# A joined row of block a placed one group sooner on VectorE, and three pieces of split weights moved, in a fused attention and two-layer kernel

## The reference

```
for t in range(S):                      # batch 4, 8 heads, S = 768, D = 48
    cur = einsum(u * k[t], v[t])
    y[t] = einsum(r[t], state + cur)
    state = w[t][..., None] * state + einsum(k[t], v[t])
x = rows of y as 3072 tokens x 384
xn = x / sqrt(mean(x*x) + 1e-6) * rms_g
x1 = (silu(xn @ w_gate) * (xn @ w_val)) @ w_out          # 384 -> 1536 -> 384
out = (s * relu(x1 @ w_in)**2 + b) @ w_out2              # 384 -> 2048 -> 384
```

## Time and profile before

| | |
|---|---|
| time, median of 3 runs | 1005.98 us (1005.86 to 1006.84) |
| the profiled execution | 1004.6 us, of which the span from first to last instruction is 1002.8 us |
| busy, of the span | PE 98%, DVE 56%, ACT 33%, POOL 27% |
| granted TensorE clock | mean 0.985; 1.00 of full speed in the stretch from 60 us to 604 us |
| stage 1 | about 60 us to 160 us of the span |
| stages 2 to 5 | about 94 us each, 160 us to 540 us |

### The profile page before, as it was taken

How to read it: one execution, slowest core, us unless ns; L and a number is a source line. 1 busy time by engine, 2 the same in 40 slices (tenths; PEclk the granted TensorE clock), 3 DMA queues, 4 the chain that set the end, 5 groups by cost and what they waited for, 6 DMA issues and landing times.

```text
span 1002.8 us, 23059 instructions
## 1 busy us (share of the span) xinstructions
PE 982.6 (98%) x9704; PEld 818.8 (82%) x9704; DVE 560.8 (56%) x783; ACT 331.9 (33%) x570; POOL 270.9 (27%) x199
## 2 busy tenths in 40 slices
PE   7888999999999999999999999999999999999998
PEld 7877788888888878888888888888888888888898
DVE  7799967774866487558743225506236054161440
ACT  1452324233323323242323445405225053160340
POOL 4654624362644346234600650000000000000000
PEclk7799999999999999999999999999999999999999
DMA  7380243117013601440126201021020110201000
GB/s 283 111 330 3 91 148 111 38 56 226 33 50 104 198 2 49 159 142 3 49 62 233 69 16 64 1 32 32 11 52 0 21 42 10 52 0 21 12 8 24
DMA packets 70779, 73.97 MB, mean 74 GB/s; under 512 B 50465, under 2 KB 55073, under 8 KB 69409
## 3 DMA queue, kind: packets, MB, share of 16 engines
q1 hardware_dynamic: 70112, 71.52, 22.5%
q10 hardware_dynamic: 576, 1.14, 0.3%
HBM read 59.27 MB, written 13.37 MB: 72 GB/s over the span
## 4 chain that ended last, share of the span: by engine, by line
PE 85%; DVE 9%; issue 4%; ACT 1%; POOL 0%; DMA 0%; DVEq 0%; ACTq 0%; POOLq 0%
PE value_o_ps L676 12%; PE mix_gate_ps L676 12%; PE o_ps L1598 11%; PE level_ps L47 10%; PE o_ps L688 8%; PE mix_gate_ps L1598 5%; PE mix_gate_ps L47 5%; PE value_o_ps L47 5%; PE value_o_ps L688 4%; DVE K L1035 3%; PE level_ps L624 2%; PE mix_gate_ps L624 2%; PE o_ps L1611 2%; PE level_ps L511 2%; DVE near L1075 2%
## 5 line engine op out<-in xcount | busy, mean ns | idle before, releaser
L1372 POOL TENSOR_TENSOR R<-R,arena 128x512 f32<-128x512 f32 x72 | 110.3, 1545 | 179.1 <-PE level_ps L511 81.8
L1697 DVE SCALAR_TENSOR_TENSOR sqr<-relu,sb_col 128x512 f32<-128x512 f32 x96 | 72.3, 753 | 73.2 <-ACT relu L1659 73.2
L1214 DVE TENSOR_TENSOR u_raw<-value_o_ps,u_raw 128x512 f32<-128x512 f32 x66 | 45.4, 688 | 98.6 <-PE value_o_ps L676 98.6
L909 ACT ACTIVATE u_hi<-u_raw 128x512 fp32r<-128x512 f32 x66 | 41.7, 632 | 163.6 <-DVE u_raw L1214 163.6
L902 ACT ACTIVATE u_raw<-mix_gate_ps 128x512 f32<-128x512 f32 x72 | 43.0, 597 | 146.7 <-PE mix_gate_ps L676 146.7
L676 PE MATMUL mix_gate_ps<-x_hi,w_hi 128*128 128x512 f32 x216 | 85.4, 396 | 0.5 <-DVE w_lo L1199 0.5
L676 PE MATMUL value_o_ps<-x_hi,w_hi 128*128 128x512 f32 x216 | 85.8, 397 | 0.0
L676 PE MATMUL value_o_ps<-x_hi,w_lo 128*128 128x512 f32 x216 | 84.2, 390 | 0.0
L676 PE MATMUL mix_gate_ps<-x_hi,w_lo 128*128 128x512 f32 x216 | 84.2, 390 | 0.0
L676 PE MATMUL mix_gate_ps<-x_lo,w_hi 128*128 128x512 f32 x216 | 84.2, 390 | 0.0
L676 PE MATMUL value_o_ps<-x_lo,w_hi 128*128 128x512 f32 x216 | 84.1, 389 | 0.0
(11 more groups left out here) (221 smaller groups left out, 2351.4 us busy)
## 6 DMA issues: line engine op xcount, KB each, us to landing
kr_nat<-kr SPq DMA_DIRECT2D x10, 1152.0 KB, 5.8
K<-kT SPq DMA_DIRECT2D x12, 512.0 KB, 4.3
arena<-wT SPq DMA_DIRECT2D x12, 512.0 KB, 6.3
R<-rT SPq DMA_DIRECT2D x10, 512.0 KB, 3.9
w_raw<-wgv SPq DMA_DIRECT2D x12, 384.0 KB, 5.4
v_sb<-v SPq DMA_DIRECT2D x12, 384.0 KB, 4.3
x_scratch<-x_sb SPq DMA_DIRECT2D x18, 256.0 KB, 2.3
x_raw<-x_scratch SPq DMA_DIRECT2D x6, 768.0 KB, 4.5
```

The lines of the kernel that those rows point to most:

```text
L1214: dve.tensor_tensor(u[:, f % 2], value_ps[:], u[:, f % 2], ALU.mult).then_inc(u_done, 1)
L1372: pool.tensor_tensor(q, q, decay(blk, l, 0), ALU.mult).then_inc(rmul_done, 1)
L1697: dve.scalar_tensor_tensor(out=sq[f % 2][:], in0=relu[f % 2][:], scalar=sb_col[:, 0:1], in1=relu[f % 2][:], op0=ALU.mult, op1=ALU.mult).th ...
```

## The change

The tables change, and one use of them. The placing of block a's joined middle row on DVE gets its own table and moves from behind group 7 to behind group 6 in all stages from 1 on. PE's table is not changed. Of stage 1's split weights, wo_lo piece 1 moves from group 7 to 6, and w_lo of f = 8 from group 17 to 19. Because the tables are read in a fixed order inside one group, u_lo of f = 2 now stands behind the moved work.

```
 LOWER_AT, MIDDLE_AT = (3, 5), (7, 9)
+MIDDLE_PLACED_AT = (6, 9)
...
-LATE_WEIGHTS = (5, 8, 9, 11, 14, 17, 20, 23, 28)
-LATE_OUT = (7, 13, 16, 25, 27)
+LATE_WEIGHTS = (5, 8, 9, 11, 14, 19, 20, 23, 28)
+LATE_OUT = (6, 13, 16, 25, 27)
...
-            if k in MIDDLE_AT:
-                blk = MIDDLE_AT.index(k)
+            if k in MIDDLE_PLACED_AT:
+                blk = MIDDLE_PLACED_AT.index(k)
                 place_middle(s, blk)
                 advance_third(s, blk)
```

## The result

| | before | changed |
|---|---|---|
| median of 12 runs | 1006.04 us (1003.1 to 1007.78) | 1003.81 us (1002.17 to 1004.82) |
| ratio to before | | 0.9978, 95% interval 0.9970 to 0.9986 |
| profiled execution | 1004.6 us, span 1002.8 | 1003.75 us, span 1002.0 |

The account below looks back on a forecast made before the run. PE is busy almost throughout, so DVE's order is worth at most PE's 4.8 us of waits. -1.1 + 0 - 0.7 = -1.8 us takes 1005.98 to 1004.2 us; own range 1003.8 to 1004.7, 8 in 10 from 1003.0 to 1005.9 us.

Parts of the forecast that it names:

- Stages 2 to 5: Sooner copies of block a's middle row end PE's wait at the joined matmuls: 0.27 us a stage, -1.1 us.
- the idle bracket: PE's idle time shown for the copy wait in stages 2 to 5: 0.21 us a stage, the lower bound.
- Stage 1, groups 6 and 7: DVE and POOL take turns, so the new order ends at the same 87.6 us: 0 us.
- the copy wait: PE's wait for block a's middle row; its 0.34 us piece before `out 2` becomes more wait for u_lo.
- w_lo, -0.7 us: Moving w_lo of f = 8 ends PE's 0.76 us keys wait in stage 1; first `attend` starts 0.7 us sooner.
- The idle in stage 1: Rival: DVE's 0.76 us idle in groups 6 and 7 comes back; -2.6 us, 1003.4 us, chance 0.19.
- the later stages: Rival: stages 2 to 5 give nothing, another wait ending just behind the copies; -0.7 us, 1005.3 us, chance 0.12.
- second turn: Rival: POOL takes two turns in a row ahead of stage 1's u_lo; -0.1 us, 1005.9 us, chance 0.07.
- the states were not made late: Rival denied here: moved w_lo makes stage 1's state sums late; +0.3 us, 1006.3 us, chance 0.07.
- the first rival: DVE's 0.76 us idle in stage 1 comes back, `out 2` starts sooner; 1003.4 us, chance 0.19.

Follow-up runs that it names:

- the part alone: Changed kernel with w_lo of f = 8 back at group 17: distance 525.95 us, 1.10 us less than before, ratio 0.9985.
- w_lo alone: Kernel before with only w_lo of f = 8 moved from group 17 to 19: distance 526.27 us, 0.78 us less, ratio 0.9997.
- POOL held: Changed kernel with POOL's three natural products of stage 1 kept back until DVE has made w_lo of f = 4: distance 523.39 us, ratio 0.9953.
- the states first: Changed kernel with w_lo of f = 9 and 10 made behind the state sums: 526.90 us, ratio 0.9989; run again 524.81 us.
- the old order with POOL held: Kernel before with POOL's three natural products of stage 1 kept back until DVE has made w_lo of f = 4: distance 527.17 us, one run.
- The filled wait: Changed kernel with identity matmuls, results unused, where PE waits at `out 2` in stage 1: distance 529.39 us, ratio 1.0038.

## Why the prediction came out as it did

The forecast was 1004.2 us, and 1003.81 us was measured. The forecast difference was 1.8 us. The distance shows 1.87 us, the timed runs 2.2 us (1.4 to 3.0). By its steps:

- **Stages 2 to 5, -1.1 us.** Right. The distance between joined matmuls fell from 5.67 to 5.39 us, and the part alone gives 1.10 us. Taking the difference of distances (0.27 us) and not the idle bracket (0.21 us) was worth 0.2 us of accuracy. u_lo had 1.7 us of slack, as worked out.
- **Stage 1, groups 6 and 7, 0 us.** Right, and for the reason given. The key quarter, wo_lo and u_lo end 0.28, 0.82 and 0.55 us behind POOL's instructions, where I had 0.30, 0.81 and 0.54 us. `out 2` starts 7.22 us behind u (7.30 us before), gate 4 still waits 0.5 us, and the bracket at `out 2` grew by the 0.3 us of the copy wait. With POOL's three products away, the same change of order makes wo_lo and u_lo ready 1.1 us sooner.
- **w_lo, -0.7 us.** The amount is right, and partly by luck: the first `attend` starts 47.07 us behind u, before 47.76 us, so 0.69 us. The path is right, since the state sum is what `attend` then starts behind, but two terms were off by 0.2 us and cancel. I had the state sum 0.26 us later, and it is 0.07 us later (46.86 against 46.79 us). w_lo did end 0.82 us behind POOL, where I had 0.81 us, but POOL's products began some 0.2 us sooner than I had them. And I let `attend` start at the very end of the sum. It starts 0.21 us behind it (47.07 against 46.86 us), and 0.20 us behind it with w_lo alone and with POOL held. That the state sum set the start is shown by the run with the states first, where the sum ends 1.0 us sooner and `attend` starts 0.27 us sooner.
- **Rivals.** The idle in stage 1 did not come back, the later stages gave what they should, POOL took no second turn, and the states were not made late. With POOL's products out of the way the idle does come back, as the first rival has it.
- **The chances.** I gave 0.59 to less than 0.2% and 0.35 to more. The ratio of 0.9978 is just beyond, with an interval over both, so this is not decided. The span forecast for the profiled execution (1001.0 us) missed by 1.0 us because stage 0 was longer in it.

## What to carry to other kernels

An idle stretch on the engine that is waited for is worth filling only when what it delays would not have been held anyway. Here, in groups 6 and 7 of stage 1, each VectorE instruction with two SBUF inputs was held to the end of a GpSimd instruction, and swapping them permuted the turns and saved nothing. Beside VectorE instructions that read PSUM, GpSimd work cost VectorE nothing, so place the two by what they read. Measure a gain of 1 to 2 us in 1000 by the distance between two events in the traces, with the parts alone adding up to the whole, before believing a median of runs that spread by 3 us or more. Look at the granted clock inside the distance first, since one fall of it was worth more than the whole change.

## What the runs showed of the hardware

In the first execution with the states first, PE stood idle for 2.59 us at `out 2`, and the clock it was then granted was 0.50 (1.2 GHz), against 1.00 (2.4 GHz) before. Its matmuls of 512 columns started 0.43 us apart instead of 0.23 us. In order of time:

```profile
87.86 0.80 PE L689 MATMUL o_ps<-u_hi,wo_hi 128*128 128x512 f32 x1 [2.59 <-DVE u_lo L1223]
88.46 0.63 PE L689 MATMUL o_ps<-u_lo,wo_hi 128*128 128x512 f32 x1
88.89 0.63 PE L689 MATMUL o_ps<-u_hi,wo_lo 128*128 128x512 f32 x1
```

The same happened in the old order with POOL held, behind an idle of 2.08 us, where the fall is seen after the second matmul:

```profile
96.73 0.50 PE L688 MATMUL o_ps<-u_hi,wo_hi 128*128 128x512 f32 x1 [2.08 <-DVE u_lo L1222]
...
97.36 0.63 PE L688 MATMUL o_ps<-u_hi,wo_lo 128*128 128x512 f32 x1
```

It did not happen behind the 2.27 us of the earlier trace rows, nor behind the 2.2 and 2.3 us of the two parts alone, nor behind the 2.6 and 2.5 us of the two executions of the changed kernel and the 2.6 us of the second one with the states first. So the same program has it in one execution and not in another, and it costs 2.1 us in the distance (526.90 against 524.81 us). The Trainium skill (TensorE: Matmul & The Clock Gate, Part 1: The HAM clock gate) says that a gate sets the engine's clock to 1.2 or 2.4 GHz by how busy it has been; the two levels and an idle stretch ahead of each fall agree with it. That a wait of 2 us or more in stage 1 (at `out 2` or `out 3`) was followed by a fall in some executions is what these two show. That the wait was the cause is not shown. How often it happens is open, and so is whether the change, which made that wait 0.3 us longer, made it more frequent. The mean clock of whole executions gives no sign of that: the execution with the fall has 0.981 and the next one 0.986, but over the 12 runs of the changed kernel it averages 0.985, and over the runs of the kernel before 0.984 to 0.985. The filled wait was meant to tell and was sized wrongly.

The second is PE's idle of 1.39 and 1.91 us without any engine to wait for, in stages 2 and 3, when instructions were put in front of them in stage 1. The changed kernel has none of that kind of any length there. The first matmul of `attend` in stage 2 to that of stage 3 took 96.20 us instead of 94.63 us, and from stage 3 to stage 4 95.67 us instead of 93.56 us. I took no run that tells what it comes from.
